# Wider, padded attention tiles in a fused linear-attention and two-layer MLP kernel

## What is computed

```
for t in range(S):
    state = alpha[:, :, t, :, None] * state + einsum('bhd,bhe->bhde', k[:, :, t], v[:, :, t])
    y[:, :, t] = einsum('bhd,bhde->bhe', q[:, :, t], state)
```

## Time and profile before

| | us |
|---|---|
| median of three runs | 899.65 |
| the profiled execution's own time | 901.47 |
| its span, first to last instruction | 899.6 |
| TensorE busy | 889.0 |
| first `hidden` matmul starts | 30.21 |

### The profile page before, as it was taken

One profiled execution on the slowest core, in us unless ns is written; L12 is line 12 of the kernel. 1 busy time (PEld: TensorE's weight loads), 2 busy tenths in 40 slices (PEclk: granted clock), 3 DMA queues, 4 the chain that ended last, 5 costly groups with the idle time before them and its releaser, 6 DMA issues.

```text
span 899.6 us, 12721 instructions
## 1 busy us (share of the span) xinstructions
PE 889.0 (99%) x5042; PEld 735.4 (82%) x5042; DVE 316.8 (35%) x500; ACT 336.9 (37%) x600; POOL 308.5 (34%) x244
## 2 busy tenths in 40 slices
PE   8899999999999999999999999999999999999998
PEld 7788888888888888878888888888888888888886
DVE  7576444335425443452234431221121211211211
ACT  3654343333333343433344543333333433433332
POOL 1644243333424432433333333333333333333232
PEclk9999999999999999999999999999999999999999
DMA  9813111111220311110033200000000000000001
GB/s 266 286 46 87 47 45 46 45 45 45 73 56 5 88 47 45 45 45 10 1 105 100 76 1 0 36 1 1 36 0 1 36 1 0 36 1 1 36 0 37
DMA packets 19421, 42.18 MB, mean 47 GB/s; under 512 B 3248, under 2 KB 9648, under 8 KB 19360
## 3 DMA queue, kind: packets, MB, share of 16 engines
q1 hardware_dynamic: 19360, 41.34, 15.6%
HBM read 34.65 MB, written 4.72 MB: 44 GB/s over the span
## 4 chain that ended last, share of the span: by engine, by line
PE 96%; DMA 2%; SPq 1%; issue 0%; ACT 0%
PE h_ps L767 44%; PE o_ps L780 44%; PE att_ps L685 2%; PE att_ps L719 2%; DMA w_out_raw<-w_out 2%; PE att_ps L722 2%; PE att_ps L695 1%; PE att_ps L739 1%; SPq L277 0%; SPq L283 0%; ACT x_parts L412 0%; SPq L300 0%; ACT inputs L450 0%; ACT k_tok L405 0%; SPq L279 0%
## 5 line engine op out<-in xcount | busy, mean ns | idle before, releaser
L368 POOL TENSOR_TENSOR g_parts<-h_act,g_parts 128x512 fp32r<-128x512 f32 x192 | 252.3, 1314 | 563.1 <-ACT g_parts L437 563.1
L780 PE MATMUL o_ps<-g_parts,w_out_hi 128*128 128x512 f32 x1152 | 327.1, 389 | 0.0
L767 PE MATMUL h_ps<-x_parts,w_in_hi 128*128 128x512 f32 x1152 | 297.5, 393 | 0.5 <-ACT x_parts L412 0.5
L780 PEld LDWEIGHTS o_ps<-g_parts,w_out_hi 128*128 128x128 f32 x1152 | 216.3, 188 | 45.0
L767 PEld LDWEIGHTS h_ps<-x_parts,w_in_hi 128*128 128x128 f32 x1152 | 213.0, 188 | 45.4 <-issue 0.7
L437 ACT ACTIVATE g_parts<-h_act 128x512 fp32r<-128x512 f32 x192 | 121.3, 632 | 290.0 <-PE o_ps L780 238.5
L579 DVE SCALAR_TENSOR_TENSOR h_act<-h_ps,h_gate 128x512 f32<-128x512 f32 x96 | 66.4, 691 | 290.5 <-ACT h_gate L432 290.5
L780 PE MATMUL o_ps<-g_parts,w_out_lo 128*128 128x512 f32 x576 | 165.6, 389 | 0.0
L767 PE MATMUL h_ps<-x_parts,w_in_lo 128*128 128x512 f32 x576 | 161.9, 389 | 0.0
L576 DVE SCALAR_TENSOR_TENSOR h_act<-h_gate,h_ps 128x512 f32<-128x512 f32 x96 | 65.6, 683 | 185.0 <-ACT h_gate L429 185.0
L767 PEld LDWEIGHTS h_ps<-x_parts,w_in_lo 128*128 128x128 f32 x576 | 108.1, 188 | 22.8
(11 more groups left out here) (100 smaller groups left out, 386.3 us busy)
## 6 DMA issues: line engine op xcount, KB each, us to landing
inputs<-att_in SPq DMA_DIRECT2D x20, 673.8 KB, 5.2
w_in_raw<-w_in SPq DMA_DIRECT2D x8, 768.0 KB, 11.4
w_out_raw<-w_out SPq DMA_DIRECT2D x8, 768.0 KB, 11.8
result<-inputs SPq DMA_DIRECT2D x18, 256.0 KB, 2.3
inputs<-v_in SPq DMA_DIRECT2D x20, 192.0 KB, 5.3
x_mid<-att_in SPq DMA_DIRECT2D x3, 673.8 KB, 11.5
x_parts<-tails SPq DMA_DIRECT2D x120, 16.0 KB, 2.4
first_v<-v_first SPq DMA_DIRECT2D x4, 384.0 KB, 15.0
```

The costliest lines, as they stand in the source:

```text
L368: nc.gpsimd.tensor_tensor(g_parts[:, g % 2, 1, :], h_act[:, g % 2, :], g_parts[:, g % 2, 0, :].bitcast(F32), ALU.subtract).then_inc(g_lo, 1)
L767: last = nc.tensor.matmul(h_ps[g % 2][:, :], w[:, m, cols], x_parts[:, n % 2, part, m, :], start=m == 0 and i == 0, stop=m == KT - 1 and i ...
L780: return nc.tensor.matmul(o_ps[m][:, :], w[:, f, m * P:(m + 1) * P], g_parts[:, g % 2, part, :], start=f == 0 and w is w_out_hi and part = ...
```

## The change

The tile's rows are laid out in HBM with a pitch of 6400 bytes (`ATT_ROW`, the next multiple of 256), with keys and queries first and the decays behind them. The DMAs load all 128 partitions of a tile instead of 112; the last sixteen rows are zeros and nothing reads them. Each row of a DMA still has 6160 bytes (4096 and 2064 in the two DMAs of tile 0). The places of tiles 0 to 3 in `x_mid` are 8448 bytes (`FIRST_SLOT_W`) apart, a multiple of 256. The computations are as before, on the same 112 rows.

```diff
-ATT_W = ALPHA_W + KQ_W
+ATT_W = KQ_W + ALPHA_W
 SLOT_W = ATT_W + ALPHA_W
+LINE = 256
+ATT_ROW = -(-ATT_W * 4 // LINE) * LINE // 4
+FIRST_SLOT_W = -(-SLOT_W * 4 // LINE) * LINE // 4
...
-            return x_flat[:, t * SLOT_W:(t + 1) * SLOT_W] if t < BATCH else inputs[:, t % 2, :]
+            return x_flat[:, t * FIRST_SLOT_W:(t + 1) * FIRST_SLOT_W] if t < BATCH else inputs[:, t % 2, :]
...
-            return pairs(slot(t)[0:ROWS, 0:ALPHA_W])
+            return pairs(slot(t)[0:ROWS, KQ_W:ATT_W])
...
-            return pairs(slot(t)[0:ROWS, ALPHA_W:ALPHA_W + PAIRS * TILE])
+            return pairs(slot(t)[0:ROWS, 0:PAIRS * TILE])
...
-            return pairs(slot(t)[0:ROWS, ALPHA_W + PAIRS * TILE:ATT_W])
+            return pairs(slot(t)[0:ROWS, PAIRS * TILE:KQ_W])
...
-                first = ATT_W if t else ALPHA_W
-                sp.dma_start(slot(t)[0:ROWS, 0:first], att_in[t, :, 0:first]).then_inc(a_loaded[slot_of(t)], 16)
+                first = 0 if t else KQ_W
+                sp.dma_start(slot(t)[:, first:ATT_W], att_in[t, :, first:ATT_W]).then_inc(a_loaded[slot_of(t)], 16)
                 if t == 0:
-                    sp.dma_start(slot(t)[0:ROWS, first:ATT_W], att_in[t, :, first:ATT_W]).then_inc(kq_loaded, 16)
+                    sp.dma_start(slot(t)[:, 0:first], att_in[t, :, 0:first]).then_inc(kq_loaded, 16)
...
-    att = np.zeros((TILES, 2, HALF, ATT_W), np.float32)
+    att = np.zeros((TILES, 2, HALF, ATT_ROW), np.float32)
...
-    att = np.ascontiguousarray(att.reshape(TILES, P, ATT_W)[:, 0:ROWS, :])
+    att = att.reshape(TILES, P, ATT_ROW)
```

More of the change, by code:

```diff
@@ L514, in make_decays @@
                 dve.wait_ge(seeded, 2 * t + 1)
-                loaded = slot(t)[0:ROWS, 0:ALPHA_W]
+                loaded = slot(t)[0:ROWS, KQ_W:ATT_W]
                 nc.vector.tensor_tensor_scan(slot(t)[0:ROWS, ATT_W:SLOT_W], loaded, seeds[:, :], 0.0, ALU.mult,
@@ L1062, in lay_out @@
     decays[:, :, 0:HD, :, 1:] = alpha[..., ::-1]
-    att[..., 0:ALPHA_W] = decays.reshape(TILES, 2, HALF, ALPHA_W)
-    att[:, :, 0:HD, ALPHA_W:ALPHA_W + PAIRS * TILE] = k[..., ::-1].reshape(TILES, 2, HD, PAIRS * TILE)
-    att[:, :, 0:HD, ALPHA_W + PAIRS * TILE:] = q.reshape(TILES, 2, HD, PAIRS * TILE)
-    att = np.ascontiguousarray(att.reshape(TILES, P, ATT_W)[:, 0:ROWS, :])
+    att[:, :, 0:HD, 0:PAIRS * TILE] = k[..., ::-1].reshape(TILES, 2, HD, PAIRS * TILE)
+    att[:, :, 0:HD, PAIRS * TILE:KQ_W] = q.reshape(TILES, 2, HD, PAIRS * TILE)
+    att[..., KQ_W:ATT_W] = decays.reshape(TILES, 2, HALF, ALPHA_W)
+    att = att.reshape(TILES, P, ATT_ROW)
     v = np.asarray(inputs["v"]).reshape(BATCH, HEADS, CHUNKS, TILE, HD)[:, :, :, ::-1, :]
```

## The result

The changed kernel takes 898.45 us (median of 12 runs, 898.05 to 898.93) against 900.3 us of the kernel before measured beside it (12 runs, 898.37 to 902.91): a ratio of 0.998, 95% interval 0.997 to 0.9989. (The ratios are estimated from the runs of both kernels and can differ a little from the quotient of the two medians.) It is faster, by 1.0 to 2.7 us, and more even: its runs spread over 0.9 us, those of before over 4.5.

A forecast was written before the change was run, and what follows sets the result against it. Late loads in the opening were taken as the only shortenable part; 1.12 us from weight waits plus 1.4 from tile 1 made 2.5, so 899.65 - 2.5 = 897.1 us, own range 896.6 to 897.8, full range 896.4 to 899.8.

The forecast's parts named there:

- What bounds the kernel: Whole span: TensorE is busy 851.74 of 851.75 us from 43.75 on, so only the opening can be shortened.
- issue and computation: All engines: same DMAs in the same order, same instructions on the same 112 rows, so 0 us.
- One load: DMA engines, opening: a 6160-byte row falls from 400 to 243 ns, a tile from 2.8 to 1.94 us.
- Tile 1: VectorE's first wait: tile 1 there at 7.5 to 9.1, taken 8.3, its scan 1.4 us earlier (0.7 to 2.2).
- the cap of 1.9: Opening: tile 1's earlier scan counts only up to about 1.9 us, limited by `warm_up` ending at 12.23.
- Rival A: Tile 1 comes no earlier, only the two weight waits go: 898.5 us; chance 20%.
- The two weight quarters: ScalarE's waits for first `w_in` and `w_out` quarters vanish, worth 0.72 and 0.40 of 3.28 us idle: 1.12 together.
- The sum: Opening gains 1.12 + 1.4 = 2.5 us, subtracted from the 899.65 median: 897.1 us; forecast's chance 60%.
- its signs: Opening: no ScalarE idle before its first two splits, near 400 GB/s, tile 1's scan 7.6 to 9.1, loop 27.3 to 28.4.
- B: Slow rate has another origin and improves just enough to pay for the eighth row: 899.65 us; chance 10%.
- C: Rows stay slow at 400 ns and there are more of them: 901.1 us (900.6 to 901.8); chance 10%.
- The 358 GB/s of HBM that were weighed: Loads, by a skill rule: rows would take 275 ns, tile 1's gain be 0.2 smaller, the time 897.4.

The follow-up runs named there:

- last two versions: Changed kernel with GpSimd scaling tile 4's keys and queries one step sooner (898.79 us, ratio 0.9988), then with only the keys moved (897.82 us, ratio 0.9968).
- before, second: The kernel before, unchanged, profiled again: 901.36 us, span 899.6.
- before, third: The kernel before, unchanged, profiled a third time: 899.95 us, span 898.2.
- before, fourth: The kernel before, unchanged, profiled a fourth time: 900.13 us, span 898.3.
- wide tiles 0 and 1: Changed kernel with 128 rows loaded for tiles 0 and 1 only, 112 for the others: 898.95 us, ratio 0.9988.
- aligned, 112 rows: Changed kernel (pitch 6400, keys first, aligned places) with 112 rows loaded instead of 128: 899.85 us, ratio 0.999.
- `w_out` split later: Kernel before with ScalarE's split of the first `w_out` quarter moved behind `first_state(3)`, loads unchanged: 901.57 us, ratio 1.0014.
- two halves: Changed kernel with each tile loaded as two DMAs of 64 rows: 903.92 us (4 runs), ratio 1.0044.
- rows-alone: Kernel before with 128 rows loaded per tile; pitch, order and places as they were: 898.66 us, ratio 0.9972.

## Why the prediction was right, and where its sizes were off

**What bounds the kernel** and **issue and computation**: right in what they put at nothing. The loop behind the opening took 869.4 to 869.9 us in every profile of the kernel before and the changed one.

**One load**: right, on the value taken: 406 GB/s were assumed and 394 and 411 measured in the two profiles; a row was put at 243 ns and its packet takes 235.

**Tile 1**: the range of 7.5 to 9.1 held, and so did both ends of its lag of 0 to 1.4 us: landing at 1.72 + 5.1 = 6.8 in the first profile and 1.72 + 6.6 = 8.3, the very value taken, in the second. In the first it came before VectorE was free, so G, by which tile 1's scan starts earlier, was 9.79 - 7.67 = 2.12, over the cap of 1.9. The cap used the time at which `warm_up` ended before; in the first profile of the changed kernel TensorE's first 32 filling matmuls took 6.06 us instead of 6.67. That is no effect of the change: over all profiles, of either kernel, they took 5.4 to 6.7 us, and why is open. Rival A (tile 1 no earlier) is out.

**The two weight quarters**: the waits went as forecast (the first `w_out` quarter landed at 6.00 + 13.7 = 19.7, where 19.9 was worked out), and the sum of what they are worth was too small. The profiles obey one line. Where nothing waits for a weight quarter and the clock stays up, the loop starts 19.06 us after tile 1's scan: 7.67 to 26.73, 8.36 to 27.42, 8.12 to 27.17, 7.84 to 26.90, and in the last two versions 8.50 to 27.55 and 8.05 to 27.11; 8.26 would give 27.32. Against that line:

| profile | scan of tile 1 | line | loop start | excess |
|---|---|---|---|---|
| before, first | 9.79 | 28.85 | 30.21 | 1.36 |
| before, second | 9.86 | 28.92 | 29.73 | 0.81 |
| before, third | 9.12 | 28.18 | 28.77 | 0.59 |
| before, fourth | 8.84 | 27.90 | 28.51 | 0.61 |
| wide tiles 0 and 1 | 8.26 | 27.32 | 27.87 | 0.55 |
| aligned, 112 rows | 10.21 | 29.27 | 30.57 | 1.30 |
| `w_out` split later | 10.06 | 29.12 | 30.44 | 1.32 |
| two halves | 10.84 | 29.90 | 32.37 | 2.47 |

The excess of the first is the term that the record sized at 1.12. It missed 0.24 of it: the first `hidden` also waits for VectorE's low part of tile 2 (the wait beside L747, which the description ahead of the prediction leaves out), late because ScalarE's high part was (TensorE's idle time before that matmul is 0.23 us now and was 0.46). The rows from the second to "wide tiles 0 and 1", with no wait for `w_in`, give `w_out` alone: 0.55 to 0.81 us, where the record had 0.40, though ScalarE's idle time for it is 3.2 to 3.4 us in all of them. The next two rows have no such wait; theirs is the clock's fall, 1.3 us. The last has both, 3.79 us of waiting for `w_out` and the fall.

**The sum**: its terms were the right ones and its base was not. In the first profiles the opening gained 2.12 + 1.36 = 3.48 us where 2.5 were forecast, and the medians gained 1.85 and, beside the second profile, 1.45 (900.06 to 898.61). The step that failed is "so I subtract from the median": terms read from an execution of 901.47 us belong to that execution. At the median (profiles three and four) the waits are shorter: the scan at 9.0 instead of 9.79, and no wait for `w_in`. There it is 28.64 - 27.1 = 1.6 us, with 27.1 the mean of the changed kernel's two, and that is what the medians say. The 899.65 of three runs was itself 0.65 below the 900.3 of twelve. The two errors, terms too small for the execution that they were read from and an execution slower than the median, partly cancelled, and that is luck: with the 3.48 us that the first profiles show, the same subtraction would have given 896.2, under the full range. The time came out 1.35 above the forecast, outside its own range of 896.6 to 897.8 and inside the full one. By the record's own measure, in which faster meant below 897.85, it lies among the times to which it gave 0.34, though twelve runs of each kernel do tell it from no change. Of its signs, the loop start of 27.3 to 28.4 was met in the second profile (27.42) and not in the first (26.73).

**Rivals B and C** fall with the window of 411 GB/s. But C's question, rows or alignment, was the right one to leave open: the rows-alone and alignment-alone kernels answer it. The 358 GB/s of HBM that were weighed (the Trainium skill, DMA: Bandwidth & Descriptors, "Where 436 GB/s comes from") do not hold this kernel back: 411 GB/s over 12 us, with one core running.

What stays open: why a few engines land tile 1 late in most profiles, up to 1.7 us behind the others with 128 rows and about 2 with 112.

## What to carry to other kernels

Load tiles over all 128 partitions in one DMA, even if rows are filling: here 14% more bytes went at 1.6 times the rate, and what was queued beside them gained too. An idle time of 3.2 us in the chain was worth 0.6 because the next condition stood right behind it; write down what is late next before pricing a wait. And before subtracting terms of one profile from a median, ask whether that profile lies at the median: profile a second time where runs spread by more than the gain.

## What the runs showed of the hardware

- While tiles of 112 partitions, or of two times 64, were being loaded in the opening, the busy DMA engines moved 246 and 242 GB/s against 411 with 128 partitions. A packet of 6160 bytes took a median of 392 and 442 ns against 235, and a packet of 3072 bytes of a 128-partition transfer in flight with them 211 and 215 against 121. Alignment of rows and places to 256 bytes showed 270 GB/s against 246 in one profile of each, and 247, 273 and 249 in three more without it; by packets, 343 ns against 369 to 398. So some help to the slow loads is not excluded, and nothing is certain; with 128 partitions a packet took 235 ns either way.
- The granted TensorE clock fell from 2.4 to 1.2 GHz in the three profiles in which TensorE had stood idle longest before the attend of tile 0 (1.95, 2.21 and 2.88 us), and in two of them, with no other wait, it cost 1.3 us of opening; after 1.59, 1.71 and 1.79 us of idle time there, in three profiles of the kernel before, it did not fall. Late loads therefore probably cost twice in some runs of the kernel before: the twelve beside the experiments with a mean clock of 0.998 or less took 901.3 to 904.8 us, the others 898.4 to 903.2. None of the twelve has a profile.
- VectorE's two-input split in SBUF took 1.75 us when it started before GpSimd's tensor work, which then took 2.07 us instead of 1.28, and 3.95 when it started after it. In these rows the two take turns: whichever started later ends 1.1 to 1.6 us after the other, 0.1 us less than it takes alone.
